# Attention inside a three-stage kernel: probabilities normalised before the value product, values as weights, one transpose less per unit

## The chip, the core and the metric

One core of a Trainium2 chip runs one program. The metric is the device time in microseconds of one execution; lower is better. The kernel before was run three times: 1199.18 us is the median, 1197.22 the lowest, 1200.24 the highest. One further execution was taken by the hardware profiler; all rows come from it.

## What is computed

Chunked attention with 8 memory keys, then two feed-forward networks over the 3072 tokens. Cut to what matters:

```python
# q, k, v: (4, 8, 768, 64); mem_k, mem_v: (4, 8, 8, 64); all float32
for c in range(24):                              # chunks of 32 queries
    keys = concat(mem, k[l_start:r_end])         # 8 + up to 56 keys: 16 left, 32 own, 8 right
    scores = (q_c @ keys.T) / 8
    a = exp(scores - max(scores))
    a = a / (sum(a) + 1e-9)
    out[c] = a @ values                          # same 64 positions
x = out.transpose(0, 2, 1, 3).reshape(3072, 512)
x = (sigmoid(x @ w_gate) * (x @ w_val)) @ w_out  # 512 -> 1536 -> 512, network A
h = x @ w_in                                     # 512 -> 2048, network B
out = (rational(h)) @ w_out2                     # 2048 -> 512
```

## The kernel before, in words

Tokens are cut into 6 tiles of 128 positions (NT) times 4 batch rows (B). A **unit** is one tile of one batch row with all 8 heads: 24 units. Eight units make one super-block, of which there are three (NS). For each super-block the kernel does attention of its 8 units, then network A over the block's 1024 tokens with a seven-product scheme (`chain`, with sums and snapshots between the products). Network B comes last, in six blocks (from about 668 us on). Each float32 product of the networks is made of three products of values split in a high and a low part; the splits are copies on ScalarE (high) and subtractions on VectorE (low). Attention itself uses plain float32 products, which show as two passes each in the trace.

**A unit before.** `scores` (line 1081): 32 small products, 64 rows deep, with a 64x32 tile of queries as weights and 64 keys streaming, for 4 head pairs, 4 chunks and 2 heads; the two heads of a pair use the two halves of the rows and write two different PSUM banks. VectorE `softmax` (731) takes the row maximum and subtracts it into SBUF; ScalarE `exp_scores` (401) takes the exponential. TensorE `turn(g, True)` (1093) transposes four 128x128 matrices, ScalarE `copy_turned` (406) copies the result to SBUF, and `weigh_values` (1104) makes 32 small products with a 64x32 tile of transposed exponentials as weights and 65 columns streaming: 64 of values and one of ones, which gives the sum. VectorE `normalize` (742) adds 1e-9 to that sum, takes the reciprocal and multiplies it in while it moves the output to SBUF. `turn(g, False)` transposes that output a second time, and ScalarE `stage_x` (413) copies it into x_raw, tokens along the columns, as network A wants it. Keys and values that lie outside the sequence have zero values and a zero in the column of ones.

**What sets the order.** Every engine has a queue written out by hand: `attention` exists once for TensorE (1205), VectorE (886) and ScalarE (540), and works through pairs of units a, b. Between their steps `at(p, place)` puts splits of weights and tokens on VectorE (917, 945) and ScalarE (567, 597), and `fill()` puts other products on TensorE. In the first stretch a fill is three 128x128 products of the identity (`warm_up`, 1118), six passes. In the two later stretches a fill is a third of an output product of network A (`third`, 1165), four products with 512 columns. There are 36 thirds to do there: 30 lie inside attention, 6 behind it. After attention `last_operands` (556 and 899) makes sums and splits of the last tokens, with an activation table load on ScalarE; the first `chain` (1122) waits for them, for the snapshots of its own first product and for `x_staged`.

**Loads.** SyncE issues all transfers (238 to 375), in one queue in order. Queries and keys of unit g wait for the scores of g-2, values for the value products of g-2; one load of values carries 4 x 4 x 65 columns a row. Output weights of network A (`load_oraw`) go through three buffers. GpSimd only makes weight sums.

Line numbers: scores L1087, transposes L1100, value products L1112, warm-up L1120, products of a third L1188 to L1202, of a chain L1152 to L1159; VectorE L735 and L738 (softmax), L746, L748, L750 (normalize), L809 (chain sum); ScalarE L404 (exponential), L410 and L420 (the copies), L455 (snapshot).

## Time and profile before

| | |
|---|---|
| median of 3 runs | 1199.18 us (1197.22 to 1200.24) |
| the profiled execution | 1198.92 us, its span in the trace 1196.6 us |
| TensorE (PE) busy | 1168.5 us, 98% of the span |
| VectorE (DVE) busy | 904.0 us, 76% |
| ScalarE (ACT) busy | 751.8 us, 63% |
| granted TensorE clock | 0.998 of full on the mean |
| first attention stretch | about 5 to 61.9 us |
| second (middle) | 207.1 to 269.9 us |
| third (middle) | 419.4 to 482.2 us |

PE is TensorE's products, PEld its weight loads, which overlap the products. A busy PE is not a PE at its peak, since products are pipelined and a recorded duration holds latency: what a group of products costs is read from the start of one group to the start of the next. "issue" stands where an engine waited for nothing that the profile shows.

### The profile page before, as it was taken

To read this page: it belongs to the slowest core of one execution; us is meant where nothing else is said; L and a number is where in the kernel's file an instruction comes from. 1 tells how busy PE (TensorE), PEld (TensorE's weight loads), DVE (VectorE), ACT (ScalarE), POOL (GpSimd) and SP (SyncE) were. 2 spreads that over 40 slices of the span, in tenths; PEclk is the share of its full clock that TensorE was granted. 3 is DMA by queue.
4 is the path that set the end of the run, shared out by engine and by line. 5 is a ranking of instruction groups with operands and counts; after the bars stand their busy time and mean duration, and the time that the engine had idled before them with its cause. 6 is when DMAs were issued, how large, how long until landed. Compare 5 with 4: busy or idle time off the path is not lost.

```text
span 1196.6 us, 21070 instructions
## 1 busy us (share of the span) xinstructions
PE 1168.5 (98%) x8160; PEld 957.1 (80%) x8160; DVE 904.0 (76%) x1387; ACT 751.8 (63%) x1224; POOL 120.7 (10%) x150
## 2 busy tenths in 40 slices
PE   8899999899999998999999999999999999999998
PEld 7778888677888866788887888888888888888887
DVE  3686566567666655776558899998998998988987
ACT  2465555455555544555556787877877877877875
POOL 2122322002322200232300000000000000000000
PEclk9999999999999999999999999999999999999999
DMA  8411411742241174332208300200200200200000
GB/s 281 156 53 65 156 54 53 259 144 79 98 168 53 54 256 137 106 132 81 88 18 290 132 1 1 71 1 1 71 0 0 70 0 0 70 0 0 36 1 35
DMA packets 40720, 97.79 MB, mean 82 GB/s; under 512 B 4288, under 2 KB 4288, under 8 KB 40640
## 3 DMA queue, kind: packets, MB, share of 16 engines
q1 hardware_dynamic: 40640, 96.68, 23.6%
q8 instruction: 55, 0.90, 0.3%
q14 instruction: 25, 0.20, 0.1%
HBM read 84.09 MB, written 12.58 MB: 81 GB/s over the span
## 4 chain that ended last, share of the span: by engine, by line
PE 57%; DVE 1%; DMA 1%; SPq 0%; issue 0%; ACT 0%; ACTq 0%
PE ps_h L1263 7%; PE ps_h L1258 7%; PE ps_h L1259 7%; PE ps_y L1302 7%; PE ps_y L1298 7%; PE ps_y L1296 7%; PE ps_h L1152 3%; PE ps_h L1159 3%; PE ps_h L1154 3%; PE ps_y L1197 1%; PE ps_y L1202 1%; PE ps_y L1198 1%; DMA oraw<-wo_l 1%; PE ps_y L1188 0%; PE ps_y L1292 0%; PE ps_y L1290 0%
## 5 line engine op out<-in xcount | busy, mean ns | idle before, releaser
L1152 PE MATMUL ps_h<-xop,wop 128*128 128x512 f32 x504 | 197.2, 391 | 2.9 <-DVE x_raw L809 2.6
L1154 PE MATMUL ps_h<-xop,wop 128*128 128x512 f32 x504 | 196.2, 389 | 0.0
L1159 PE MATMUL ps_h<-xop,wop 128*128 128x512 f32 x504 | 155.9, 390 | 0.0
L1258 PE MATMUL ps_h<-x_split,weights 128*128 128x512 f32 x384 | 149.4, 389 | 0.0
L1259 PE MATMUL ps_h<-x_split,weights 128*128 128x512 f32 x384 | 149.4, 389 | 0.0
L1296 PE MATMUL ps_y<-weights,hid 128*128 128x512 f32 x360 | 140.0, 389 | 0.0
L1298 PE MATMUL ps_y<-weights,hid 128*128 128x512 f32 x360 | 140.0, 389 | 0.0
L788 DVE TENSOR_TENSOR wop<-rawp,wop 128x448 fp32r<-128x448 f32 x144 | 90.9, 660 | 56.6 <-ACT wop L441 56.5
L809 DVE TENSOR_TENSOR x_raw<-ps_h,probs_t 128x512 f32<-128x512 f32 x72 | 49.5, 688 | 87.0 <-PE ps_h L1159 86.6
L675 ACT ACTIVATE tmp<-ps_h 128x512 f32<-128x512 f32 x96 | 57.2, 595 | 92.4 <-PE ps_h L1263 92.4
L1152 PEld LDWEIGHTS ps_h<-xop,wop 128*128 128x128 f32 x504 | 94.6, 188 | 25.3 <-DVE x_raw L809 4.3
L1154 PEld LDWEIGHTS ps_h<-xop,wop 128*128 128x128 f32 x504 | 94.7, 188 | 20.0
L1159 PEld LDWEIGHTS ps_h<-xop,wop 128*128 128x128 f32 x504 | 94.6, 188 | 19.8
L1197 PE MATMUL ps_y<-hid,wout 128*128 128x512 f32 x264 | 107.0, 405 | 2.6 <-issue 1.9
L1198 PE MATMUL ps_y<-hid,wout 128*128 128x512 f32 x264 | 103.9, 394 | 0.0
L1263 PE MATMUL ps_h<-x_split,weights 128*128 128x512 f32 x384 | 102.6, 389 | 0.0
L1302 PE MATMUL ps_y<-weights,hid 128*128 128x512 f32 x360 | 96.2, 389 | 0.0
L1007 DVE TENSOR_TENSOR tmp<-tmp 128x512 f32<-128x512 f32 x96 | 66.2, 689 | 30.5 <-ACT tmp L678 30.5
L483 ACT ACTIVATE hid<-x_raw 128x512 fp32r<-128x512 f32 x72 | 45.4, 630 | 64.8 <-DVE x_raw L823 64.8
L1259 PEld LDWEIGHTS ps_h<-x_split,weights 128*128 128x128 f32 x384 | 72.1, 188 | 15.0
L1263 PEld LDWEIGHTS ps_h<-x_split,weights 128*128 128x128 f32 x384 | 72.1, 188 | 14.9
L1258 PEld LDWEIGHTS ps_h<-x_split,weights 128*128 128x128 f32 x384 | 72.0, 188 | 14.9
(89 smaller groups left out, 2254.4 us busy)
## 6 DMA issues: line engine op xcount, KB each, us to landing
rawp<-wgv_l SPq DMA_DIRECT2D x36, 512.0 KB, 3.5
oraw<-wo_l SPq DMA_DIRECT2D x72, 256.0 KB, 3.7
unit<-v_l SPq DMA_DIRECT2D x24, 520.0 KB, 5.8
unit<-k_l SPq DMA_DIRECT2D x24, 512.0 KB, 5.7
unit<-q_l SPq DMA_DIRECT2D x24, 256.0 KB, 4.4
x_stage<-y_dram SPq DMA_DIRECT2D x6, 1024.0 KB, 6.0
out<-stage SPq DMA_DIRECT2D x24, 256.0 KB, 2.2
braw<-wb_l SPq DMA_DIRECT2D x11, 512.0 KB, 5.5
```

Source lines behind the costliest of these rows:

```text
L788: nc.vector.tensor_tensor(wop[:, c % 2, 1, cols], rawp[:, c % 2, 256 + 448 * i:256 + 448 * (i + 1)], wop[:, c % 2, 0, cols].bitcast(F32), ...
L1152: nc.tensor.matmul(dst, w_h[k], xop[:, m, 0, k, :], start=first and k == 0, stop=False, skip_group_check=True)
L1154: nc.tensor.matmul(dst, w_l[k], xop[:, m, 0, k, :], start=False, stop=False, skip_group_check=True)
L1159: last = nc.tensor.matmul(dst, w_h[k], xop[:, m, 1, k, :], start=False, stop=k == 1, skip_group_check=True)
L1197: nc.tensor.matmul(ps_y[:, m, :], w_at(0, m), h[0], start=f == 0, stop=False)
L1198: nc.tensor.matmul(ps_y[:, m, :], w_at(1, m), h[0], start=False, stop=False)
L1258: nc.tensor.matmul(dst, lhs(c, 0), x_split[:, 0, c, :], start=(c == 0), stop=False)
L1259: nc.tensor.matmul(dst, lhs(c, 1), x_split[:, 0, c, :], start=False, stop=False)
L1263: last = nc.tensor.matmul(dst, lhs(c, 0), x_split[:, 1, c, :], start=False, stop=(c == KT - 1))
L1296: nc.tensor.matmul(ps_y[:, m, :], hid_b(i, 0)[:, P * m:P * (m + 1)], wb_at(i, 1, 0), start=(i == 0), stop=False)
L1298: nc.tensor.matmul(ps_y[:, m, :], hid_b(i, 0)[:, P * m:P * (m + 1)], wb_at(i, 1, 1), start=False, stop=False)
L1302: nc.tensor.matmul(ps_y[:, m, :], hid_b(i, 1)[:, P * m:P * (m + 1)], wb_at(i, 1, 0), start=False, stop=False)
```

## The change

The probabilities are cleared outside the sequence (first and last tile), summed, and multiplied by the reciprocal of their sum plus 1e-9 in SBUF, before they are transposed. The value product has the values as weights (64 rows by 64 columns) and the transposed probabilities streaming (32 columns), so that its output has tokens along the columns. The second transposes are gone; `stage_x` copies from PSUM bank 1 of the unit. Both heads of a pair write that one bank, on different halves of the partitions. The column of ones is gone. The order of the queues is written anew: on TensorE nine fills lie in a pair of units, seven in the last, and two before the last value product (36 in all, none behind attention); the transposes of unit b and its value product move into the next pair.

```diff
             def stage_x(g):
                 b, s, n = g % 2, g // UNITS, g % UNITS
-                act.wait_ge(xturn_done, g + 1)
+                act.wait_ge(pv_done, g + 1)
...
-                                     ps_att[b][:, 0, :].rearrange("p (h n) -> p h n", h=HP),
+                                     ps_att[b][:, 1, :].rearrange("p (h n) -> p h n", h=HP),
...
             # ScalarE, attention
                     a, b = first + 2 * p, first + 2 * p + 1
+                    if p:
+                        copy_turned(b - 2)
                     exp_scores(a)
+                    at(p, 0)
                     if p:
                         stage_x(b - 2)
                     copy_turned(a)
-                    at(p, 0)
+                    at(p, 1)
                     exp_scores(b)
-                    at(p, 1)
-                    copy_turned(b)
+                    at(p, 2)
                     stage_x(a)
-                    at(p, 2)
+                copy_turned(first + UNITS - 1)
                 stage_x(first + UNITS - 1)
...
-                last_operands(s + 1, lambda place: split_wout(n + 11 + place))
+                last_operands(s + 1, between)  
...
             # VectorE
             def normalize(g):
-                b = g % 2
-                ov = ps_att[b][:, :, 0:HP * VD].rearrange("p s (h k) -> p s h k", k=VD)
-                dve.wait_ge(pv_done, g + 1)
-                nc.vector.tensor_scalar(row[b], ov[:, :, :, D], 1e-9, None, ALU.add).then_inc(den_done, 1)
-                dve.wait_ge(den_done, 2 * g + 1)
+                b, tile = g % 2, g // B
+                pr = probs[b].rearrange("p h s k -> p s h k")
+                dve.wait_ge(exped, g + 1)
+                if tile == 0:
+                    nc.vector.memset(probs[b][0:CHUNK, :, :, NMEM:NMEM + LEFT], 0.0).then_inc(cut_done, 1)
+                    dve.wait_ge(cut_done, g + 1)
+                elif tile == NT - 1:
+                    nc.vector.memset(probs[b][P - CHUNK:P, :, :, KEYS - RIGHT:KEYS], 0.0).then_inc(cut_done, 1)
+                    dve.wait_ge(cut_done, g - (NT - 2) * B + 1)
+                nc.vector.tensor_reduce(row[b], pr, AX.X, ALU.add).then_inc(den_done, 1)
+                dve.wait_ge(den_done, 3 * g + 1)
+                nc.vector.tensor_scalar(row[b], row[b], 1e-9, None, ALU.add).then_inc(den_done, 1)
+                dve.wait_ge(den_done, 3 * g + 2)
                 nc.vector.reciprocal(row[b], row[b]).then_inc(den_done, 1)
-                dve.wait_ge(den_done, 2 * g + 2)
-                nc.vector.tensor_tensor(probs[b].rearrange("p h s k -> p s h k"), ov[:, :, :, 0:D],
-                                        row[b].unsqueeze(3).to_broadcast([P, 2, HP, D]),
+                dve.wait_ge(den_done, 3 * g + 3)
+                nc.vector.tensor_tensor(pr, pr, row[b].unsqueeze(3).to_broadcast([P, 2, HP, KEYS]),
                                         ALU.mult).then_inc(norm_done, 1)
...
             # VectorE, attention
-                    if p:
-                        normalize(b - 2)
                     softmax(a)
                     at(p, 0)
-                    softmax(b)
                     normalize(a)
                     at(p, 1)
-                normalize(first + UNITS - 1)
+                    softmax(b)
+                    at(p, 2)
+                    normalize(b)
...
             # TensorE, weigh_values
                             last = nc.tensor.matmul(
-                                ps_att[b][CHUNK * c:CHUNK * (c + 1), e, VD * h:VD * (h + 1)],
+                                ps_att[b][D * e:D * (e + 1), 1, P * h + CHUNK * c:P * h + CHUNK * (c + 1)],
+                                v_sb[b][KEYS * e:KEYS * (e + 1), c, h, :],
                                 probs_t[b][KEYS * e:KEYS * (e + 1), h, CHUNK * c:CHUNK * (c + 1)],
-                                v_sb[b][KEYS * e:KEYS * (e + 1), c, h, :], start=True, stop=True)
+                                start=True, stop=True)
...
             # TensorE, attention
                     scores(a)
+                    if p:
+                        turn(b - 2)
+                    fill()
                     fill()
                     if p:
-                        turn(b - 2, False)
-                    else:
-                        fill()
+                        weigh_values(b - 2)
                     fill()
-                    turn(a, True)
+                    fill()
                     scores(b)
+                    turn(a)
                     fill()
                     fill()
                     weigh_values(a)
-                    turn(b, True)
                     fill()
-                    fill()
-                    weigh_values(b)
-                    turn(a, False)
-                    fill()
+                    if p < UNITS // 2 - 1:
+                        fill()
+                        fill()
+                turn(first + UNITS - 1)
                 fill()
-                turn(first + UNITS - 1, False)
+                fill()
+                weigh_values(first + UNITS - 1)
```

The rest of the diff moves with it: SyncE's queue in the first stretch asks for keys of unit g before values of g-1, in the middle stretches for output weights three to four places earlier; ScalarE's and VectorE's `at_start` and `at_middle` spread the same splits over three places a pair, with the splits of output pieces n+11 to n+13 moved up by one; `softmax` waits for the transposes of unit g-2 in place of the second ones; the host no longer appends the column of ones.

## Rows read from the trace of the kernel before

**Rows 1.** Windows, busy us (and instructions) of each engine, clock, DMA share, GB/s.
```profile
5.00:61.90 56.90, 48.97 (x1293) 43.35 (x1293) 30.77 (x57) 22.75 (x38) 9.47 (x12) 0.97 0.63 212
207.10:269.90 62.80, 57.14 (x1235) 43.78 (x1235) 38.35 (x71) 29.32 (x50) 0.00 (x0) 1.00 0.57 192
...
668.00:1196.60 528.60, 525.40 (x2318) 434.62 (x2316) 473.38 (x709) 401.33 (x612) 0.00 (x0) 1.00 0.07 24
```

**Rows 2.** TensorE's waits, first middle stretch: total us, times, longest.
```profile
PE ps_h L1100 <- ACT probs L404: 2.1, 4, 0.9
PE ps_y L1197 <- issue: 1.9, 1, 1.9
PE ps_h L1087 <- issue: 1.1, 1, 1.1
PE ps_h L1112 <- issue: 0.5, 1, 0.5
```

**Rows 3.** Lines 1112 and 1120: ns min/median/max, first and last start, forms.
```profile
L1112 PEld LDWEIGHTS ps_h<-unit,probs_t x1536: 102/106/174, 11.0 to 473.7; 64*32 64x32 f32 x192
L1112 PE MATMUL ps_h<-unit,probs_t x1536: 213/218/313, 11.0 to 473.8; 64*32 64x65 f32 x192
...
L1120 PEld LDWEIGHTS ps_y<-ident x216: 186/192/338, 1.5 to 61.8; 128*128 128x128 f32 x108
L1120 PE MATMUL ps_y<-ident x216: 275/275/580, 1.5 to 61.9; 128*128 128x128 f32 x108
```

**Rows 4.** Timeline, first attention stretch: start us, us, engine, line, what.
```profile
20.11 0.97 PE L1087 MATMUL ps_h<-unit 64*32 64x64 f32 x64
...
31.82 0.85 PE L1087 MATMUL ps_h<-unit 64*32 64x64 f32 x64
...
37.30 1.42 PEld L1120 LDWEIGHTS ps_y<-ident 128*128 128x128 f32 x12
...
38.83 0.63 PEld L1112 LDWEIGHTS ps_h<-unit,probs_t 64*32 64x32 f32 x56
...
44.49 0.93 PE L1087 MATMUL ps_h<-unit 64*32 64x64 f32 x64
...
59.49 0.60 ACT L420 ACTIVATE x_raw<-ps_h 128x512 f32<-128x512 f32 x1 [0.89 <-PE ps_h L1100]
```

**Rows 5.** Timeline, one pair of units in the second middle stretch.
```profile
452.31 1.19 PE L1202 MATMUL ps_y<-hid,wout 128*128 128x512 f32 x4
...
454.35 0.86 PE L1112 MATMUL ps_h<-unit,probs_t 64*32 64x65 f32 x64
...
455.93 0.47 PE L1197 MATMUL ps_y<-hid,wout 128*128 128x512 f32 x1
...
457.94 0.70 PEld L1112 LDWEIGHTS ps_h<-unit,probs_t 64*32 64x32 f32 x64 [0.36 <-issue]
...
458.73 0.66 PE L1100 MATMUL ps_h<-ident,probs 128*128 128x128 f32 x4
...
459.14 0.48 PE L1197 MATMUL ps_y<-hid,wout 128*128 128x512 f32 x1
...
460.25 0.83 PE L1087 MATMUL ps_h<-unit 64*32 64x64 f32 x60
```

**Rows 6.** Groups of attention, 0 to 482 us: busy us, mean ns | idle before.
```profile
L738 DVE TENSOR_TENSOR probs<-ps_h,row_stats 128x512 f32<-128x512 f32 x24 | 16.6, 692 | 0.8
...
L404 ACT ACTIVATE probs<-probs 128x512 f32<-128x512 f32 x24 | 15.1, 631 | 53.5 <-DVE probs L738 53.5
```

**Rows 7.** Timeline behind the last unit, first and second stretch.
```profile
65.18 0.50 PE L1152 MATMUL ps_h<-xop,wop 128*128 128x512 f32 x1 [0.30 <-ACT probs_t L455]
...
264.62 0.60 ACT L420 ACTIVATE x_raw<-ps_h 128x512 f32<-128x512 f32 x1
...
272.91 0.58 ACT L455 ACTIVATE probs_t<-ps_h 128x512 f32<-128x512 f32 x1
...
282.14 0.50 PE L1152 MATMUL ps_h<-xop,wop 128*128 128x512 f32 x1 [0.70 <-DVE x_raw L809]
```

More of the change, by code:

```diff
@@ L80, in build @@
         hid0 = at("hid0", 86016, [P, 2, 2, 512], F32R)
[L81 removed]
+        unit = at("unit", 94208, [P, 2, HP * P + CT * HP * KEYS + CT * HP * D])
         rawp = at("rawp", 114816, [P, 2, 2048])
@@ L288, in _ @@
             load_raw(0)
-            for p in range(1, UNITS // 2):
-                for g in (2 * p, 2 * p + 1):
-                    load_qk(g)
-                if p == 1:
+            load_qk(2)
+            for g in range(3, UNITS):
+                load_qk(g)
+                if g == 3:
                     load_raw(1)
-                for g in (2 * p, 2 * p + 1):
-                    load_v(g)
+                load_v(g - 1)
+            load_v(UNITS - 1)
             sp.dma_start(a_raw, coef_a).then_inc(coef_loaded, 16)
@@ L319, in _ @@
                 n, g = piece_of(s, 0, TA - 2), UNITS * (s + 1)
+                load_oraw(n + 4)
                 load_qk(g + 2)
-                for ahead in (4, 5, 6):
-                    load_oraw(n + ahead)
+                load_oraw(n + 5)
+                load_oraw(n + 6)
                 load_qk(g + 3)
@@ L336, in _ @@
                 load_oraw(n + 10)
+                load_v(g + 5)
+                load_oraw(n + 11)
                 load_qk(g + 7)
                 load_v(g + 6)
+                load_oraw(n + 12)
                 load_v(g + 7)
-                for ahead in range(11, 16):
+                for ahead in (13, 14, 15):
                     load_oraw(n + ahead)
@@ L597, in at_middle @@
                 def at_middle(p, place):
-                    if p < 2 and place == 0:
-                        split_wout(n + 2 * p + 2)
-                        split_wout(n + 2 * p + 3)
+                    if p == 0 and place == 0:
+                        split_wout(n + 2)
+                        split_wout(n + 3)
                     elif p == 0 and place == 1:
@@ L736, in softmax @@
                 dve.wait_ge(max_done, g + 1)
-                wait(dve, xturn_done, g - 1)
+                wait(dve, turned_done, g - 1)
                 nc.vector.tensor_tensor(probs[b].rearrange("p h s k -> p s h k"), sc,
@@ L930, in at_start, with between @@
                     split_w(1, 1)
+            def between(place):
+                if place == 0:
                     split_w(1, 2)
-            def between(place):
-                if place == 2:
+                elif place == 2:
                     split_w(1, 3)
@@ L945, in at_middle, with between @@
                 def at_middle(p, place):
[L946 to L951 removed]
+                    if p == 0 and place == 1:
+                        split_wout(n + 2)
+                        split_wout(n + 3)
+                    elif p == 0 and place == 2:
                         copy_out_a(2 * s, 2)
                         copy_out_a(2 * s, 3)
+                    elif p == 1 and place == 0:
+                        split_w(c, 0)
+                    elif p == 1 and place == 1:
+                        split_wout(n + 4)
+                        split_wout(n + 5)
                     elif p == 1:
[L955 removed]
                         split_w(c, 1)
+                        split_wout(n + 6)
+                    elif p == 2 and place == 0:
+                        split_wout(n + 7)
                         split_w(c, 2)
+                    elif p == 2 and place == 1:
+                        split_w(c, 3)
+                        split_wout(n + 8)
                     elif p == 2:
[L959 removed]
                         split_x(s + 1, B11)
[L961 removed]
+                    elif p == 3 and place == 0:
+                        split_wout(n + 9)
+                        split_wout(n + 10)
+                    elif p == 3 and place == 1:
+                        token_sum(s + 1, T1, 0)
                         token_sum(s + 1, T2, 0)
+                    elif p == 3:
+                        split_wout(n + 11)
                         split_x(s + 1, B21)
[L964 removed]
+                def between(place):
+                    if place < 2:
+                        split_wout(n + 12 + place)
                 attention(UNITS * (s + 1), at_middle)
[L967 removed]
+                last_operands(s + 1, between)
             dve.wait_ge(coef_loaded, 32)
@@ L1091, in scores, with turn @@
                 last.then_inc(scores_done, 1)
-            def turn(g, first):
+            def turn(g):
                 b = g % 2
-                if first:
-                    pe.wait_ge(exped, g + 1)
-                else:
-                    pe.wait_ge(norm_done, g + 1)
+                pe.wait_ge(norm_done, g + 1)
                 for h in range(HP):
@@ L1101, in turn @@
                                                probs[b][:, h].rearrange("p s k -> p (s k)"), ident[:])
-                last.then_inc(turned_done if first else xturn_done, 1)
+                last.then_inc(turned_done, 1)
             def weigh_values(g):
```

60 lines of the change are left out of this document (25 added, 35 removed).

## The prediction, made before the change was run

> **What bounds the kernel now.** I read the busy time by stage first. TensorE is the engine on the path nearly everywhere: from 668 us to the end it is busy for 525.4 of 528.6 us, and nothing there is touched by the change [rows 1]. What the change touches is attention: a first stretch of 57 us in which only warm-up products lie between the small products, and two middle stretches of 62.8 us, in which 30 of the 36 thirds of an output product lie between them and 6 behind them. In a middle stretch TensorE is busy 57.1 of 62.8 us, VectorE 38.4 and ScalarE 29.3. So a microsecond of TensorE work added or removed there counts in full, and VectorE has room. Then the waits: in the first middle stretch TensorE waits 2.1 us for ScalarE's exponentials (what is normalised or turned too early) and 3.5 us for "issue", which no engine causes and which falls in the middle of runs of small products; I read it as instructions that come late [rows 2].
>
> **The value products: the term that decides.** Per unit there are 32 products on 64 rows, each in two passes, so 64 loads and 64 streams, before and after. Before, a weight tile is 64x32, eight fit the array side by side, and 65 columns stream. After, the weight tile is 64x64 and 32 columns stream; of the four tiles the array has room for, only the two on the diagonal are used (first half of the rows to the first half of the outputs, second to second). So each tile takes 32 passes where it took 8. What does a pass take? A load of 32 columns lasts 106 ns and one of 128 lasts 192, a stream of 65 columns 218 and one of 128 lasts 275 [rows 3]: both grow by 0.9 ns a column, the rest is latency. Twelve warm-up loads take 1.42 us, (1.42 - 0.19) / 11 = 0.112 us a pass [rows 4]. Load and stream of 128 columns at 0.9 ns each would be 0.23 one after the other, so on one tile the next load hides under the running stream, and a pass costs the longer of the two. After the change that is the load: 64 x 0.9 = 57 ns, the stream of 32 only 29. 32 passes x 0.057 = 1.8 us, and with the drain of the last (a block now takes 0.70 to its last load's end and 0.79 to what follows [rows 5]) **1.9 us instead of 0.79: +1.1 us a unit, 24 units**. Bounds: below, today's 0.79, since as many instructions are issued; if the load were as cheap per tile as the stream, 32 x 0.03 + 0.15 = 1.1. Above: load and stream in turn, 32 x 0.086 + 0.15 = 2.9; the two tiles in turn, 64 x 0.057 + 0.15 = 3.8. I take 1.9, by the 128-column row, the only one where one tile does pass after pass.
>
> The Trainium skill ("TensorE: Matmul & The Clock Gate", LDWEIGHTS) has the load cost columns / 1.2 GHz, 53 ns for 64: with it the block would be 1.8, as by the rows. The same page (Part 3, The mechanism) says that a load overlaps a running product only where the row group differs; by that rule the block would be the 2.9 above, against the warm-up row.
>
> **What goes.** The second transposes: 4 matrices a unit, 0.41 us from the block to the next product [rows 5], 24 units. And the waits: chains of a unit now have more between their links. Normalising the probabilities puts a reduction (of the maximum's size), a small add, the reciprocal and the same multiply between exponential and transpose; a VectorE operation on 128x512 takes 0.69 us. From scores to transpose: 0.69 + 0.69 + 0.63 + 0.69 + 0.4 + 0.69 [rows 6] = 3.8, some 4.4 with semaphores. TensorE's new order has four fills, a value block, a score block and a transpose in between, over 8 us in a middle stretch and 6 in the first: covered, also with VectorE's splits between. VectorE gets 8 x 0.7 = 5.6 us more per stretch, 44 of 65, costs nothing. The two clears of masked probabilities (8 of 24 units) are under 0.2 us each on VectorE, in the same cover; without it, 2 us in all. The value loads shrink by one column in 65 and are issued a little later, behind key loads; each still has a whole pair (13 us) to land. The output loads are asked for earlier, with six thirds more inside attention, but these spread over a longer stretch.
>
> **First stretch.** A pair of units after the change: scores 0.79, transpose 0.42, two fills with the mode change 1.53 (37.30 to 38.83) [rows 4], value block 1.9, fills 1.53, scores 0.79, transpose 0.42, fills 1.53, value block 1.9, three fills 2.2: 13.0 us. Before, from one pair's scores to the next: 11.7 and 12.7, and from the last pair's to the staging of the last unit (44.49 to 59.49) 15.0. After: 13.0, 13.0, and 11.65 + (0.42 + 1.53 + 1.9) = 15.5. The first pair has one value block and two transposes fewer but a fill more: -0.3. Sum **+1.8 us**.
>
> **Middle stretches.** Two fills take 2.04 us behind scores and 2.01 behind a transpose [rows 5]. A pair: 0.79 + 0.42 + 2.01 + 1.9 + 2.04 + 0.79 + 0.42 + 2.01 + 1.9 + 2.95 = 15.2. First pair without the earlier unit's transpose and value block 12.7, two of 15.2, the last with two fills fewer 13.4, then 0.42 + 2.01 + 1.9: 60.9 us to the last value block's end. The 3.5 us of late instructions stay: 64.4. Before, the last unit's staging began 57.5 us into the stretch (264.62 from 207.1) [rows 7].
>
> Now what is late next. Before, the six thirds behind attention (5.5 us) covered what follows the last unit: staging, a table load, sums, splits, snapshots. After, nothing is left to cover it: TensorE goes from the last value block into the first chain and stands before its third product about 3.7 us later, while the snapshot it needs ends 8.3 us behind the staging (272.9 + 0.6 - 264.6, less a ScalarE copy of 0.5 that leaves the queue) [rows 7]. That is a new wait of 4 to 5 us per middle stretch, and it is why I count from staging, not from TensorE's last fill: the trace of before shows TensorE held at 282.14, 17.5 us after the staging, by VectorE's sum, and in the first stretch 5.7 us after it by ScalarE's snapshot [rows 7]. So the stretch grows by what staging is later, 64.4 - 57.5 = 6.9, less one split of the output weights (0.6, VectorE's rate for this size) that leaves that queue: **+6.3 us each, 12.6 for two**.
>
> Sum: 1.8 + 12.6 = +14.4 on the profiled execution's 1198.92, which lies 0.3 below the median of 1199.18: **about 1213**.
>
> **Rivals.**
> 1. *The value block is cheap* (0.79 to 1.1): a 64-column load could be spread over both halves of its tile, or the issue of 64 pairs may bound it as now. For it: today's tile of 32 columns loads in parallel with seven others. Then at 1.1 the middle stretches come out at +6.3 - 8 x 0.8 = about 0 each, the first at -3: 1196. At 0.79: -2.6 each and -5: 1189. That is the rival on the other side. It decides where the block is under about 1.2 us.
> 2. *The block is dearer.* In turn within a tile: 24 x 1.0 more, 1237. The two tiles in turn: 24 x 1.9, 1258. Before, the two row halves wrote two banks of PSUM, now both write one. Against it: the columns of one half write one bank side by side today. The Trainium skill ("PSUM — Partial Sum Buffer", PSUM bank collisions raise a hardware error) says different row tiles can't write one bank at the same time; no row here shows that.
> 3. *Block as forecast, but the tail is covered*, or the small-product stalls shrink: 2 to 5 us less per stretch, 1203 to 1209. Or TensorE's new order makes a wait of its own (staging behind splits in ScalarE's queue, the order of loads): 1218 to 1228.
> 4. That the change doesn't do what it says: no row can show it; the transposes are visibly gone from the code.
>
> **How the numbers follow.** A difference of 0.3%, 3.6 us, is about what a measurement here tells from none. Chances: forecast 0.48, with its own range 1208 to 1219; rival 1 0.30; rival 2 0.12; rival 3 0.10. Rival 1 splits into faster (0.24) and within 0.3% (0.06); all the rest is slower. Range 1188 to 1237: it takes in rival 1 to its bound and rival 2's first price, and leaves out the two tiles in turn.
>
> **What would show it.** Right: the value products' line has 64 loads of about 130 ns in 1.8 us a block; TensorE busier by some 1.1 us a unit in attention and 0.4 less for transposes; no wait of a transpose for the exponential; a wait of 4 to 5 us in each middle stretch before the third product of the first chain. Wrong: a value block under 1.2 us, or a gap before the first chain's third product under 1 us.

## The result, and the profile after

| | before | after |
|---|---|---|
| median of the four runs | 1199.71 us (1197.22 to 1200.29) | 1215.47 us (1213.78 to 1218.38) |
| ratio | | 1.0138, 95% interval 1.0112 to 1.0164 |
| profiled execution, its span | 1198.92, 1196.6 us | 1214.59, 1212.6 us |

The changed kernel is 1.4% slower. The span grew by 16.0 us. Where that lies is read from the start of the scores of the two middle stretches, which stand at 207.48 and 419.62 before and at 207.21 and 427.76 after: **-0.3 us** up to the first, **+8.4** between them, **+7.9** from the second to the end.

TensorE's own products first: the two lines of the value products and the scores (ns min/median/max, first and last start, forms), which answer to [rows 3].

```profile
L1144 PEld LDWEIGHTS ps_h<-probs_t,unit x1536: 129/135/135, 12.4 to 491.8; 64*64 64x64 f32 x192
L1144 PE MATMUL ps_h<-probs_t,unit x1536: 219/219/241, 12.4 to 491.9; 64*64 64x32 f32 x192
L1122 PEld LDWEIGHTS ps_h<-unit x1536: 102/106/174, 5.1 to 482.0; 64*32 64x32 f32 x192
```

Each of these products shows as two passes, a load and a stream each. There are as many of both as before, with loads of 135 ns for 106. What a block costs is not in these durations. It stands in the timeline, from the start of a block to the start of what follows (first stretch, TensorE):

```profile
25.92 2.06 PE L1144 MATMUL ps_h<-probs_t,unit 64*64 64x32 f32 x64
27.91 2.27 PE L1153 MATMUL ps_y<-ident 128*128 128x128 f32 x18
...
61.90 0.48 PE L1185 MATMUL ps_h<-xop,wop 128*128 128x512 f32 x1
```

1.99 us a block, where it was 0.79 [rows 5]. All the same the first chain starts at 61.90 us, where it started before. By the windows (columns as in [rows 1], to which these lines answer) TensorE now has hardly a gap in attention:

```profile
5.00:61.90 56.90, 55.88 (x1296) 52.68 (x1297) 39.17 (x69) 22.92 (x39) 10.03 (x12) 1.00 0.63 211
207.20:271.45 64.25, 62.03 (x1202) 50.16 (x1201) 39.76 (x72) 26.33 (x46) 0.00 (x0) 1.00 0.55 182
```

It is busy for 55.9 of the first 56.9 us instead of 49.0. TensorE's waits in the whole kernel (total us, times, longest) say what went and what came:

```profile
PE ps_h L1185 <- ACT probs_t L457: 9.2, 2, 4.6
PE ps_y L1230 <- DVE wout L812: 3.7, 4, 1.5
PE ps_h L1132 <- DVE probs L770: 2.2, 4, 0.7
```

There is no wait for an exponential and none for "issue" [rows 2] (in the whole kernel before, 7.7 and 9.1 us); in their place stands 4.6 us in each middle stretch for a snapshot (L457), and up to 1.5 for the output weights' low part (L812). In the order of time, at the end of the first middle stretch:

```profile
254.77 0.50 PE L1230 MATMUL ps_y<-hid,wout 128*128 128x512 f32 x1 [1.52 <-DVE wout L812]
...
269.46 2.06 PE L1144 MATMUL ps_h<-probs_t,unit 64*64 64x32 f32 x64
271.45 0.50 PE L1185 MATMUL ps_h<-xop,wop 128*128 128x512 f32 x1
271.56 0.60 ACT L422 ACTIVATE x_raw<-ps_h 128x512 f32<-128x512 f32 x1 [3.24 <-PE ps_h L1144]
...
272.71 0.69 DVE L812 TENSOR_TENSOR wout<-oraw,wout 128x512 fp32r<-128x512 f32 x1 [6.06 <-ACT wout L450]
...
279.33 0.57 ACT L457 ACTIVATE probs_t<-ps_h 128x512 f32<-128x512 f32 x1
279.96 0.80 PE L1185 MATMUL ps_h<-xop,wop 128*128 128x512 f32 x1 [4.58 <-ACT probs_t L457]
...
289.51 0.68 DVE L828 TENSOR_TENSOR x_raw<-ps_h,probs 128x512 f32<-128x512 f32 x1
290.24 0.50 PE L1185 MATMUL ps_h<-xop,wop 128*128 128x512 f32 x1
```

The last staging (L422) starts at 271.56, 64.4 us into the stretch, the snapshot ends 8.3 us behind it, and the chain's third product starts at 279.96, after 4.58 us in which TensorE does nothing. Before, six thirds covered this time. At 290.24 TensorE takes up the product that stood at 282.14 in the kernel before [rows 7], again right behind VectorE's sum (L828), which ends at 290.19. TensorE's granted clock falls behind the gap (windows; the clock is the third figure from the end):

```profile
279.96:282.00 2.04, 2.04 (x5) 1.65 (x6) 2.04 (x3) 0.49 (x1) 2.04 (x3) 0.50 0.03 8
282.00:284.00 2.00, 2.00 (x7) 1.52 (x6) 2.00 (x3) 1.08 (x2) 0.58 (x1) 0.50 0.80 211
```

0.50 is the lower level, 1.2 GHz: a 512-column product takes 0.43 us from start to start there instead of 0.23.

### The profile page after: what moved, and what is told of

Same layout as the page of the kernel before. It is cut to its first block, busy times and chain, and to the rows that moved or that the text cites. A ratio compares the mean times of both kernels' runs of the same rounds, so it can differ in the third digit from the quotient of the medians.

```text
span 1212.6 us, 20982 instructions
## 1 busy us (share of the span) xinstructions
PE 1190.3 (98%) x8100; PEld 982.6 (81%) x8100; DVE 928.1 (77%) x1419; ACT 752.3 (62%) x1224; POOL 125.6 (10%) x150
## 4 chain that ended last, share of the span: by engine, by line
PE 93%; DVE 3%; ACT 1%; DMA 1%; issue 1%; SPq 0%; ACTq 0%; DVEq 0%
PE ps_h L1185 9%; PE ps_h L1192 9%; PE ps_h L1187 9%; PE ps_h L1298 7%; PE ps_h L1294 7%; PE ps_h L1293 7%; PE ps_y L1337 7%; PE ps_y L1333 7%; PE ps_y L1331 7%; PE ps_y L1230 5%; PE ps_y L1235 4%; PE ps_y L1231 4%; PE ps_h L1144 4%; PE ps_y L1153 2%; PE ps_h L1122 1%; PE ps_h L1132 1%
## 5 line engine op out<-in xcount | busy, mean ns | idle before, releaser
L828 DVE TENSOR_TENSOR x_raw<-ps_h,probs_t 128x512 f32<-128x512 f32 x72 | 49.4, 687 | 86.4 <-PE ps_h L1192 86.4
L807 DVE TENSOR_TENSOR wop<-rawp,wop 128x448 fp32r<-128x448 f32 x144 | 87.5, 636 | 36.3 <-ACT wop L443 36.2
```

The source lines that it names most:

```text
L807: nc.vector.tensor_tensor(wop[:, c % 2, 1, cols], rawp[:, c % 2, 256 + 448 * i:256 + 448 * (i + 1)], wop[:, c % 2, 0, cols].bitcast(F32), ...
```

## The experiments

Twelve kernels, each against the kernel before on the same chip (its medians there: 1200.66, 1200.22, 1201.56 and 1200.61 us). The changed kernel itself was run beside the first kernel only, at 1199.71, so a difference of two times from different chips can be off by what the kernel before differs by between them, up to 1.9 us. The question is threefold: what the value product costs and why; whether the rest of the change is worth anything; and what the wait behind attention costs.

### The value product: load, stream, bank

**Halves.** Each product is made as two with 32 value columns each, so that four tiles of the array are used instead of two, and twice as many instructions are issued.

```diff
-                            last = nc.tensor.matmul(
-                                ps_att[b][D * e:D * (e + 1), 1, ...],
-                                v_sb[b][KEYS * e:KEYS * (e + 1), c, h, :], ...
+                            for j in range(2):
+                                last = nc.tensor.matmul(
+                                    ps_att[b][D * e + 32 * j:D * e + 32 * (j + 1), 1, ...],
+                                    v_sb[b][KEYS * e:KEYS * (e + 1), c, h, 32 * j:32 * (j + 1)], ...
```

> The kernel after with each value product cut in two: 32 value columns as weights instead of 64, 64 products a unit instead of 32, on four tiles of 64x32 instead of two of 64x64. Everything else as after. Theory A (a tile's pass costs the longer of load and stream, and the load of 64 columns, some 57 ns, bounds it): the load is halved, a pass costs about 30 ns, 32 passes a tile as before, so a value block falls from 1.98 to about 1.1 us, about 20 us in all: 1195. Theory B (the two tiles disturb each other by writing one bank, or products are bound by their number): no change or more, a block of 2.0 to 2.6 us, 1215 to 1230. The wait of some 4.6 us before the third product of the first chain stays in both middle stretches by either.

Measured: 1237.74 us, ratio 1.0311 (1.0286 to 1.0336): 22 us slower than the changed kernel, a time that neither theory had. Two blocks of its timeline, TensorE, first stretch:

```profile
23.08 1.29 PE L1145 MATMUL ps_h<-probs_t,unit 64*32 64x32 f32 x128
24.30 1.60 PE L1155 MATMUL ps_y<-ident 128*128 128x128 f32 x12
...
27.50 0.31 PE L1122 MATMUL ps_h<-unit 64*32 64x64 f32 x6 [0.86 <-issue]
27.74 0.66 PE L1132 MATMUL ps_h<-ident,probs 128*128 128x128 f32 x4
28.24 1.50 PE L1155 MATMUL ps_y<-ident 128*128 128x128 f32 x12
29.67 1.11 PE L1145 MATMUL ps_h<-probs_t,unit 64*32 64x32 f32 x106
33.64 0.39 PE L1145 MATMUL ps_h<-probs_t,unit 64*32 64x32 f32 x22 [2.86 <-issue]
33.95 0.38 PE L1155 MATMUL ps_y<-ident 128*128 128x128 f32 x1
```

Where nothing disturbs it, the block takes 1.22 us: still 32 passes a tile, each with half the columns to load, and (1.22 - 0.15) / 32 = 33 ns a pass in place of (1.99 - 0.15) / 32 = 58, if the drain is taken as 0.15 us in both. But the next block stands still after 106 of its 128 passes. From one standstill to the next lie 6 + 4 + 12 + 106 = 128 passes. The waits of the whole kernel say that no engine is the cause:

```profile
PE ps_h L1145 <- issue: 20.6, 11, 4.0
PE ps_h L1122 <- issue: 6.1, 6, 2.3
```

The page's part on DMA queues shows the supply, in the kernel after (first line) and in this one (second):

```profile
q8 instruction: 55, 0.90, 0.3%
```

```profile
q8 instruction: 67, 1.10, 0.4%
```

Twelve packets of 16 KB more carry the 1536 more passes (a load and a stream each), 0.20 MB / 3072 = about 65 bytes an instruction, so one packet holds some 128 passes: the distance between the standstills. A block of 128 uses one up in 1.22 us. So TensorE stood for the next packet of instructions, and their supply sets how many such passes pay. That the load of 64 columns sets the pass of 58 ns is shown with the next run. What bounds a block of 1.22 us, the load of 32 columns or the number of passes, is not: in the kernel before, 8 passes a tile with 65 columns streamed would take 8 x 58 ns + 0.15 = 0.62 us by the same rule, and took 0.79.

**Half the stream.** The converse: loads of 64 columns stay, and only 16 of the 32 columns of probabilities stream.

```diff
-                                ps_att[b][..., 1, P * h + CHUNK * c:P * h + CHUNK * (c + 1)],
+                                ps_att[b][..., 1, P * h + CHUNK * c:P * h + CHUNK * c + CHUNK // 2],
...
-                                probs_t[b][..., h, CHUNK * c:CHUNK * (c + 1)],
+                                probs_t[b][..., h, CHUNK * c:CHUNK * c + CHUNK // 2],
```

> The changed kernel, with each of the 64 products with the values reading 16 of its 32 columns of probabilities: the second half of every chunk of tokens is left out of attention's output, and the loads of 64 value columns stay as they are (eight products at the start, in place of six, write the banks once). Theory A (a pass of this product takes as long as its load of weights, and what streams is hidden under it): the block stays at 1.9 to 2.0 us from its start to the next instruction's, and the total at 1212 to 1218 us. Theory B (the columns streamed set the pass, or share it with the load): the block falls to 1.0 to 1.5 us and the total to 1200 to 1208 us.

Measured: 1214.71 us (1213.08 to 1217.86), ratio 1.0102 (1.0080 to 1.0124). Timeline of TensorE:

```profile
22.31 2.04 PE L1144 MATMUL ps_h<-probs_t,unit 64*64 64x16 f32 x64
24.28 1.60 PE L1153 MATMUL ps_y<-ident 128*128 128x128 f32 x12
```

1.97 us with half the columns streamed. Theory A: what streams is hidden, and of the two only the load is left to set the pass.

**Another bank.** The second head's outputs go to PSUM bank 0 instead of 1, and the staging is two copies.

```diff
-                                ps_att[b][D * e:D * (e + 1), 1, ...],
+                                ps_att[b][D * e:D * (e + 1), 1 - e, ...],
```

> The kernel after with the second head's products written to the unit's other PSUM bank (free by then), and the staging in two copies of 64 partitions. Theory A (the load bounds the block): a block stays at 1.98 us. Theory B (row halves writing one bank take turns): a block falls to 1.0 to 1.2 us. The second ScalarE copy (0.6 us a unit) should be hidden but for the last unit of a stretch, where the staging ends 0.5 us later: +1 to +2 us in all by theory A.

Measured, in a single run: 1218.62 us. Timeline of TensorE:

```profile
26.89 2.06 PE L1146 MATMUL ps_h<-probs_t,unit 64*64 64x32 f32 x64
28.88 2.27 PE L1155 MATMUL ps_y<-ident 128*128 128x128 f32 x18
```

The block takes 1.99 us as before, so two row halves that write one bank cost nothing that these rows show. The 3 us more fit a wait before the third product, which ends behind the two copies (11.7 us in all for 9.2), but a single run can't settle so little.

### The product by itself, in the new order and in the old

**New order, old product.** The probabilities stand as weights again, 64 value columns stream, the second transposes stay out: attention's output is left with tokens along the partitions.

```diff
-                                ps_att[b][D * e:D * (e + 1), 1, P * h + CHUNK * c:P * h + CHUNK * (c + 1)],
-                                v_sb[b][KEYS * e:KEYS * (e + 1), c, h, :],
+                                ps_att[b][CHUNK * c:CHUNK * (c + 1), e, D * h:D * (h + 1)],
                                 probs_t[b][KEYS * e:KEYS * (e + 1), h, CHUNK * c:CHUNK * (c + 1)],
+                                v_sb[b][KEYS * e:KEYS * (e + 1), c, h, :],
```

> The kernel after with the value product turned back to the old orientation (transposed probabilities as 64x32 weights, 64 value columns streaming), the output left with tokens on the partitions and staged so: the second transposes and their place are not put back, so what is computed differs. All else as after. It prices the product's form alone. Theory A: a block costs 0.79 us instead of 1.98, 24 x 1.19 = 28.6 us less work for TensorE, some 2 to 4 us of it given back as new waits for copies and normalised probabilities: 1188 to 1192. The wait of 4.6 us behind attention stays. Theory B (most of the loss sits behind attention, not in the product): 1200 to 1208.

Measured: 1200.5 us, ratio 0.9993 (0.9979 to 1.0007). The step is 15 us, where 24 blocks are 28.8 us shorter: the expectation of 1188 to 1192 was missed, because almost half of the work taken out came back as waits. The time lies in theory B's range, but not for its reason (that most of the loss sits behind attention):

```profile
PE ps_h L1184 <- ACT probs_t L457: 9.6, 3, 4.6
PE ps_h L1132 <- DVE probs L770: 4.8, 6, 1.7
PE ps_h L1122 <- issue: 4.5, 5, 1.5
PE ps_y L1229 <- DVE wout L812: 4.4, 6, 1.5
PE ps_h L1144 <- issue: 2.9, 4, 1.4
```

Against the changed kernel's list, the late instructions (7.4 us) are new and the normalised probabilities cost 2.6 more. A block of 2 us had covered both. All the waits listed come to 30.7 us here and to 18.7 in the changed kernel: 12.0 of the 14.1 us that did not show.

**Old order, new product.** The kernel before, with only the value product turned and the column of ones left out of it.

```diff
-                                ps_att[b][CHUNK * c:CHUNK * (c + 1), e, VD * h:VD * (h + 1)],
+                                ps_att[b][D * e:D * (e + 1), 1, P * h + CHUNK * c:P * h + CHUNK * (c + 1)],
+                                v_sb[b][KEYS * e:KEYS * (e + 1), c, h, 0:D],
...
-                                v_sb[b][KEYS * e:KEYS * (e + 1), c, h, :],
```

> The kernel before, with its old order of units, old softmax and both transposes, and only the product with the values in the new orientation (64x64 weights, 32 columns streamed, both heads in one bank). The 65th column of the values is left out of the product, and the output's normalisation then reads numbers that are not the sums, so what it computes is something else; every instruction on the other engines keeps its size. Theory A (the block costs 1.98 us where the old one takes 0.79, and this is paid wherever TensorE is the bound): 24 x 1.19 = 28.6 us more at the most, less the waits of the old schedule that the longer blocks fill (late instructions 2.8 + 3.5 + 2.7, exponentials): 1215 to 1225 us. Theory B (the old order of units hides it no better than the new one lost it: the 14.9 us that the product alone was worth in the new order is its price in any order): 1212 to 1216 us. If the rest of the change (order, sums, one transpose less) is worth something by itself, this kernel is slower than the changed one, by up to 10 us.

Measured: 1214.72 us, ratio 1.0127 (1.0105 to 1.0150), theory B. Of TensorE's waits these are left for exponentials and for "issue", where the kernel before had 7.7 and 9.1 us:

```profile
PE ps_h L1100 <- ACT probs L404: 3.4, 7, 0.7
PE ps_h L1112 <- issue: 0.2, 1, 0.2
```

The 24 longer blocks, 28.8 us of work, thus covered 8.9 us of late instructions and 4.3 of exponentials. With both kernels the change falls into its parts (span by stage, us, from the starts of the scores in the timelines):

| | to first middle stretch | to second | to the end | span |
|---|---|---|---|---|
| before | 207.5 | 212.1 | 777.0 | 1196.6 |
| old order, new product | 213.2 | 216.6 | 781.5 | 1211.3 |
| new order, old product | 205.9 | 213.8 | 778.2 | 1197.9 |
| after | 207.2 | 220.6 | 784.8 | 1212.6 |

The product alone is worth +14.7 us in either order. These spans are of one execution each, and four runs of one kernel lie up to 4.6 us apart, so that the two agree to a tenth is luck. All the rest (24 second transposes less, normalising in SBUF, the new order) is worth +1.3 us by these spans, which is less than the runs can tell from nothing (old product: ratio 0.9993, 0.9979 to 1.0007). It gains 1.6 us (old product) or 6.0 (new) in the first stretch and loses 2.8 or 7.3 in the other two. What the transposes gave, some 24 x 0.41 = 10 us of TensorE's work, was spent there.

### What is lost behind attention

**Warm.** 20 products of the identity are put before the third product's wait in the first chain of the two later super-blocks, so that TensorE's clock stays up.

```diff
                     elif m == M6:
+                        if s and c % CHAINS == 0:
+                            for _ in range(20):
+                                nc.tensor.matmul(ps_h[:, 2, 0:P], ident[:], ident[:], start=True, stop=True)
                         pe.wait_ge(snap_done, 3 * c + 1)
```

> The kernel after with 20 dummy products of the identity (40 passes of 0.112 us, 4.5 us) on TensorE before the third product of the first chain of the second and third super-block, where it waits 4.6 us for ScalarE's snapshot. They fill the wait and should not lengthen it by more than 0.2 us. Theory A (the idle time lowers the granted clock, which stands at 0.50 for some 5 us behind the wait, and this costs some 2.5 us a stretch): the clock stays at 1.0 and the kernel is 4 to 5 us faster, 1211. Theory B (what follows the wait is bound by VectorE's sums, whatever the clock): no change.

Measured: 1217.37 us, ratio 1.0131 (1.0107 to 1.0154), theory B: no gain, with the clock at 0.998 on the mean. The clock stayed at 1.00 behind the filled waits, and in part the wait moved on to VectorE's sums (1.5 us of these waits in the changed kernel). The longest, in the first middle stretch, lowered the clock in its turn:

```profile
PE ps_h L1188 <- DVE x_raw L828: 4.3, 4, 2.2
```

```profile
291.66 0.50 PE L1188 MATMUL ps_h<-xop,wop 128*128 128x512 f32 x1 [2.16 <-DVE x_raw L828]
```

```profile
291.66:293.70 2.04, 2.04 (x6) 1.62 (x7) 0.54 (x1) 1.21 (x2) 0.00 (x0) 0.62 0.49 129
```

So raising the clock behind the gap brings nothing here: TensorE at full speed meets a VectorE that started late. It doesn't say that a low clock is free where nothing else binds.

**Output weights first.** VectorE stood 6.06 us for ScalarE's part of the output weights n+12 (see the timeline above), with the last tokens' splits and sums queued behind it; ScalarE's part was queued behind the staging. It moves before it, in the middle stretches: the new place splits n+12, and the old one behind the staging, `between(0)`, is empty.

```diff
                     exp_scores(b)
                     at(p, 2)
                     stage_x(a)
                 copy_turned(first + UNITS - 1)
+                if first:
+                    at(UNITS // 2, 0)
                 stage_x(first + UNITS - 1)
```

> The changed kernel, with ScalarE's split of the output weights n+12 moved in the two middle stretches from behind the staging of the last unit to before it. VectorE's splits of T2 and T1 stand behind its own half of those weights and waited 6 us for ScalarE's half. Theory A (the chain's third product waits for the snapshot, the snapshot waits for T3's sum on VectorE, and VectorE started 3 us late because of the weights): the wait of 4.6 us before the third product falls to 1 to 3 us and TensorE's clock stays at its upper level or falls for less time; 4 to 8 us less in all, 1207 to 1212 us. Theory B (what bounds is ScalarE's own queue behind the staging, T3 and T4's parts and the snapshot): the wait changes by under 0.7 us each, 1214 to 1217 us. Moved too far up, the weights' split waits for a piece that TensorE has not read yet and the staging gets later: 1218 us or more.

Measured: 1207.16 us, ratio 1.0062 (1.0038 to 1.0087): 8.3 us less than the changed kernel (9 by the ratios), theory A. Its wait before the third product, in both middle stretches together:

```profile
PE ps_h L1189 <- ACT probs_t L457: 3.7, 2, 1.9
```

**And the snapshot first.** ScalarE's snapshot goes ahead of its parts of T2 and T1.

```diff
                 split_x(s, T4, 0)
+                snapshot(2 * NQ * s, 0)
                 split_x(s, T2, 1)
                 split_x(s, T1, 1)
```

> As the run before, and ScalarE's snapshot of the next super-block's first product moved up, ahead of its parts of T2 and T1 for the second half of the tokens. Theory A: the snapshot comes some 2 to 3 us earlier, the wait before the third product is under 1 us; but ScalarE's part of T2 and T1 then comes a microsecond later, and what follows waits for VectorE's sums. 0 to 4 us less than the run before: 1204 to 1211 us. Theory B (VectorE's sums bound what follows): the time of the run before, and waits for VectorE in the chain grow by what this one loses.

Measured: 1209.37 us, ratio 1.0075 (1.0051 to 1.0099): 2 us more than without, which the intervals don't tell from none, so theory B and no gain. The snapshot's wait is gone. 1.7 us for T2 and T1's low parts have come, and the waits for VectorE's sums have grown from 1.7 to 3.7:

```profile
PE ps_h L1191 <- DVE x_raw L834: 3.7, 4, 1.7
...
PE ps_h L1198 <- DVE xop L805: 1.7, 3, 0.7
```

**Four thirds kept behind attention.** The other way to fill that time.

```diff
                     fill()
-                    fill()
+                    if not (first and p >= 2):
+                        fill()
                     scores(b)
...
                     if p < UNITS // 2 - 1:
                         fill()
-                        fill()
+                        if not (first and p >= 1):
+                            fill()
```

> The changed kernel, with four of the 36 thirds of output pieces that stand between the units of a middle stretch left out there, so that four are left behind attention, ahead of the first chain (six stood there in the kernel before, none in the changed one). Theory A (the forecast's new wait: the snapshot comes 8.3 us behind the staging, and nothing is left on TensorE to fill that time): 4 x 1.05 = 4.2 us of the wait of 4.6 are filled, its clock does not fall, and both middle stretches give back 4 to 6 us: 1203 to 1208 us. Theory B (these thirds only covered other waits between the units, or the ring of three pieces of output weights keeps VectorE and with it the snapshot back by the same time): waits for DVE wout or for turned probabilities grow, and the total is 1212 to 1218 us.

Measured: 1212.98 us, ratio 1.0121 (1.0092 to 1.0150), in theory B's range, but by a wait that neither theory named. The wait for the snapshot fell from 9.2 to 1.9 us and that for output weights from 3.7 to 0.9, but late instructions took their place:

```profile
PE ps_h L1122 <- issue: 7.8, 5, 2.3
PE ps_h L1185 <- DVE x_raw L828: 2.7, 4, 0.8
PE ps_h L1185 <- ACT probs_t L457: 1.9, 2, 1.0
```

The thirds between the units had a use that no list of waits of the changed kernel shows. As I read it, long products give the supply time to bring the next packet of small ones.

**Output weights n+9 as well.** On top of "output weights first", VectorE's split of n+9 moves ahead of the seventh unit's softmax, which waits for scores: a new place 3 in the third pair holds it, in place of place 0 in the fourth.

```diff
                     normalize(b)
+                    if first:
+                        at(p, 3)
```

> As tail1 (the output weights n+12 split before the last staging), and VectorE's split of the output weights n+9 moved from behind the softmax of the seventh unit to before it. TensorE waited 1.5 us for it in each middle stretch, at 254.77 in the changed kernel. Theory A (that wait is on the path and the split has room before the softmax): it goes, 2 to 3 us less than tail1: 1204 to 1206 us. Theory B (the ring of three pieces holds it back, or the softmax and with it the normalised probabilities come later by as much): the wait stays or moves to the turns, 1206 to 1210 us.

Measured: 1203.39 us (10 runs), ratio 1.0025 (1.0009 to 1.0040): 3.8 us less again, theory A and a little more. What is left of the waits in the middle stretches (two of the four for normalised probabilities lie in the first stretch), and the clock behind the gap:

```profile
PE ps_h L1193 <- ACT probs_t L457: 3.7, 2, 1.9
PE ps_h L1140 <- DVE probs L774: 2.2, 4, 0.7
```

```profile
273.90:275.70 1.80, 0.00 (x0) 0.00 (x0) 1.80 (x3) 1.80 (x5) 1.80 (x2) 1.00 0.00 0
275.70:278.00 2.30, 2.29 (x10) 1.90 (x11) 2.30 (x4) 1.12 (x3) 0.39 (x1) 1.00 0.06 20
```

The same wait of 1.9 us is there, and the clock stays at 1.00. In the run "output weights first" it was 0.76 and then 0.50 behind the first of its two waits of this length, and 1.00 behind the second. This may be part of the 3.8 us; but the waits for output weights fell from 4.2 to 0.6 us over the whole kernel, which leaves it little. No run tried it alone. Nor did the clock stay up each time: over the ten runs it was 0.995 to 1.000 on the mean, with 1205.93 and 1206.12 us in the two at 0.995 and 1201.69 in the one at 1.000, which is the one in the trace. One at 0.998 took 1206.68, so the clock isn't all of that spread.

**The last two** leave one third less between the units in the first two pairs only (two thirds then stand behind attention), and the second of them also moves n+13's split behind the snapshot.

```diff
                     if p < UNITS // 2 - 1:
                         fill()
-                        fill()
+                        if not (first and p < 2):
+                            fill()
```

> As tail3 (output weights n+12 and n+9 split earlier), and one third of an output piece left out behind the values of the first and of the third unit of each middle stretch, so that two thirds stand behind attention. Theory A (early in the stretch the supply of instructions has slack, so that no wait for issue appears as it did where four were left out, and the wait of 1.86 us before the chain's third product is filled): 2 to 4 us less than tail3, 1199 to 1202 us, about the kernel before. Theory B (waits for issue or for VectorE's weights take its place): 1203 to 1207 us.

> As tail4, and ScalarE's split of the output weights n+13 moved behind the snapshot of the chain's first product, so that the snapshot starts 0.5 us earlier in both middle stretches. Theory A: where a wait before the third product is left, 0.5 us less each, 1198 to 1202 us. Theory B (nothing is left of that wait, or the weights now come late for TensorE): the time of tail4 within 1 us, or waits for VectorE's output weights behind the third product.

Measured: 1203.08 us and 1202.96 us (12 runs each), ratios 1.0025 (1.0010 to 1.0039) and 1.0025 (1.0010 to 1.0040). Theory B in both. In the first of them the wait for the snapshot is gone altogether, and this line has come:

```profile
PE ps_h L1130 <- issue: 3.7, 4, 1.3
```

3.7 us for 3.7 us, and 0.7 more of late instructions in a value block. No version of the changed kernel that was tried beats the kernel before. The best three are level with one another and 0.25% slower than it, with intervals that begin at 1.0009 and 1.0010.

## Why the prediction was right, point by point

Predicted 1213 us, measured 1215.47: right in sign, in size and in its main mechanism, the value block. That the sum came so near is in part luck, since its smaller terms were wrong in opposite directions: 2.1 us too many in the first stretch, 3.7 too few in the other two, and within a middle stretch 3.5 us of late instructions that went against about as much that it didn't have.

- **The value block**, predicted 1.9 us, measured 1.99. Halving the load brought the pass from 58 to 33 ns, halving the stream did nothing: on these tiles a pass costs the longer of load and stream, and that is the load, 57 ns by [rows 3] and 58 measured. Rival 1 is refuted by the block's length, rival 2 by the same and by the run with two banks. The Trainium skill's figure ("TensorE: Matmul & The Clock Gate", LDWEIGHTS) of 53 ns for 64 columns agrees to 5 ns; the rule of its Part 3, The mechanism, that a load overlaps a running product only where the row group differs, does not hold for these passes on one tile: it gave 2.9. The same section lets a load run ahead also where it goes to a background weight buffer; these loads may be such, which no row shows.
- **"The 3.5 us of late instructions stay": wrong.** They are gone, in all three stretches. The term was mis-sized by its whole length, and with it the claim that a microsecond of TensorE's work counts in full: the product costs 14.7 us net for 28.8 us of work, since the longer blocks cover 8.9 us of late instructions (old order, whole kernel).
- **First stretch**, predicted +1.8, measured -0.3 to the next stretch's start. All of it is in the first pair: the second pair's scores start at 16.97 us where they started at 20.11, 3.1 us earlier, and the prediction had 0.3 for that pair. 2.6 us of issue wait at 14.30 us, which no row of the prediction held, went, and with it the lower clock behind it: the stretch's granted clock is 1.00 instead of 0.97 [rows 1].
- **Middle stretches**, predicted +6.3 each, measured +8.4 and +7.9. The last staging came 64.4 us into the stretch, which is the number predicted, but by other parts, and so by luck: no late instructions, and instead 1.5 us for the output weights, 0.7 for the normalised probabilities and 0.7 for eight blocks of 1.99. The wait for output weights was missed: the prediction noted that the loads are asked for earlier and never asked where VectorE's split of them stands in its queue. The prediction took the stretch before from 207.1, where its scores start at 207.48: the staging is 7.2 us later, not 6.9. The rest lies behind the staging. TensorE met VectorE's sum 18.7 us behind it, then 17.4, where it was 17.5 and 17.2 before and the prediction took 0.6 off for a split that leaves the queue; nothing came off. In the first of the two stretches four VectorE operations ahead of that sum (278.51 to 283.1) take 1.2 us each instead of 0.7, while GpSimd makes weight sums; whether that is the cause no run tried.
- **The new wait** before the third product was predicted at 4 to 5 us, twice: measured 4.58 and 4.58, with the snapshot 8.3 us behind the staging. What the prediction took as given is that it has to be so long. 2.7 us of it went when VectorE no longer waited for ScalarE's half of one output piece; that and n+9's split are worth some 12 us of the 16.
- **Normalising is covered**: nearly. The transposes waited 2.2 us in four places, 0.7 at most. The exponentials' waits went, as predicted.

## What to carry to other kernels

With small products, ask which operand is loaded more often than it is used: with a load before every product, a pass on one tile cost its weight columns where these were more than the columns streamed. Splitting the load over more tiles made the undisturbed block shorter, streaming fewer columns did not. When work is taken from or given to the bounding engine in a schedule with small waits in it, expect less than all of it at the surface (here half), and price each wait by what would follow if it went. After moving work across a stage's end, look in every engine's queue for an operation without a hurry that stands ahead of the ones that have it: one split moved up by one place gave back more here than any other step.

## What the runs showed of the hardware

- **Instruction supply is a bound of its own.** It shows as waits for "issue" in or just ahead of runs of small products, wherever these come too densely: 9.1 us with blocks of 0.79 us in the kernel before, none listed in the changed kernel with 1.99 us, 29 us with 128 passes a block, 7.8 us when four thirds of long products were taken from between the blocks of each middle stretch. Instructions came in packets of 16 KB, about 128 passes with their loads, and between two of the standstills lay 128.
- **The clock fell to its lower level behind both gaps of 4.6 us in the changed kernel (0.50, and 0.54 in the second), behind one of four gaps of 1.9 us in two others, and behind one of 2.2 us in "Warm" (0.62).** In the kernel before it was 0.66 behind the wait of 2.6 us at 14.30 us. Filling the gap of 4.6 us with idle products kept the clock up behind it and gained nothing, since another engine bounded what followed.
- **Two row halves writing one PSUM bank** ran at the pace of two banks, 1.99 us a block in both. The Trainium skill ("PSUM — Partial Sum Buffer", PSUM bank collisions raise a hardware error) has it that different row tiles can't write one bank at the same time, and reports the error as measured where both write the same 32 partitions of it. Here the halves write different partitions, and no run showed an error or a delay.
